# Splitting the first batch's queries and keys straight from PSUM, on ScalarE and VectorE

## What is computed

```python
def _attn_ref(q, k, v, n_sink, window):          # q, k, v: (2, 8, 768, 64), n_sink 4, window 128
    scores = 1.0 / np.sqrt(D) * np.matmul(q, k.transpose(0, 1, 3, 2))
    keep = (pos[None, :] < n_sink) | ((rel >= 0) & (rel < window))
    scores = np.where(keep, scores, -1000000000.0)
    a = np.exp(scores - np.max(scores, axis=-1, keepdims=True))
    a = a / (np.sum(a, axis=-1, keepdims=True) + 1e-09)
    return np.matmul(a, v)

def _moe_ref(x, U, V, w_ch1, w_ch2):             # rank 32, 512 -> 2048 -> 512
    u = x + (x.transpose(0, 2, 1) @ U @ V).transpose(0, 2, 1)
    return u + np.maximum(u @ w_ch1, 0.0) @ w_ch2

def _moe2_ref(x, w_tok1, w_tok2, w_ch1, w_ch2):  # 768 -> 256 -> 768, 512 -> 1536 -> 512
    u = x + (np.maximum(x.transpose(0, 2, 1) @ w_tok1, 0.0) @ w_tok2).transpose(0, 2, 1)
    return u + np.maximum(u @ w_ch1, 0.0) @ w_ch2
```

## Time and profile before

| | |
|---|---|
| median of three runs | 656.0 us (655.68 to 656.14) |
| the profiled execution | 657.41 us |
| its span, first to last instruction | 655.6 us |
| around the span | 1.8 us |
| PE busy | 631.2 us, 96% of the span |
| GpSimd busy | 367.0 us, 56% |
| DVE busy | 336.7 us, 51% |
| ACT busy | 316.2 us, 48% |
| attention of batch 0 | 3.9 us to about 77 us |

### The profile page before, as it was taken

One profiled execution on the slowest core, in us unless ns is written; L12 is line 12 of the kernel. 1 busy time (PEld: TensorE's weight loads), 2 busy tenths in 40 slices (PEclk: granted clock), 3 DMA queues, 4 the chain that ended last, 5 costly groups with the idle time before them and its releaser, 6 DMA issues.

```text
span 655.6 us, 10345 instructions
## 1 busy us (share of the span) xinstructions
PE 631.2 (96%) x3532; PEld 565.9 (86%) x3532; DVE 336.7 (51%) x733; ACT 316.2 (48%) x707; POOL 367.0 (56%) x373
## 2 busy tenths in 40 slices
PE   6888999999999999999999999999999999999998
PEld 5878888889888987799999988889998888899986
DVE  7776552433333254276757562186758325676411
ACT  4655575455444553464545444364544445554321
POOL 8544366656464656246656745375656543757262
PEclk9998999999999999999999999999999999999999
DMA  8344244433324425223232243233232343431142
GB/s 182 85 93 113 50 129 118 110 102 108 97 67 107 148 65 146 64 67 110 81 106 88 70 135 101 81 112 97 81 108 87 103 136 98 134 94 47 49 130 95
DMA packets 88276, 65.51 MB, mean 100 GB/s; under 512 B 43008, under 2 KB 72192, under 8 KB 88224
## 3 DMA queue, kind: packets, MB, share of 16 engines
q1 hardware_dynamic: 88224, 64.85, 35.0%
HBM read 61.42 MB, written 3.15 MB: 98 GB/s over the span
## 4 chain that ended last, share of the span: by engine, by line
PE 87%; DVE 5%; ACT 3%; POOL 2%; issue 2%; DMA 0%; DVEq 0%; ACTq 0%; POOLq 0%
PE bank L1356 33%; PE bank L1155 21%; PE bank L1322 10%; PE bank L1212 4%; PE bank L1185 4%; PE bank L1193 3%; PE bank L1286 3%; PE bank L1249 2%; PE bank L1230 2%; PE bank L1170 1%; PE bank L1263 1%; POOL w_lo L753 1%; ACT w_hi L774 1%; PE bank L1348 1%; DVE x_nat L978 1%
## 5 line engine op out<-in xcount | busy, mean ns | idle before, releaser
L753 POOL TENSOR_TENSOR w_lo<-w_raw,w_hi 128x512 fp32r<-128x512 f32 (+1 forms) x158 | 205.9, 1309 | 170.5 <-ACT w_hi L774 170.0
L774 ACT ACTIVATE w_hi<-w_raw 128x512 fp32r<-128x512 f32 (+1 forms) x158 | 96.3, 618 | 61.0 <-PE bank L1356 43.0
L1155 PE MATMUL bank<-b_hi,a_hi 128*128 128x384 f32 x280 | 94.8, 338 | 1.0 <-DVE temps L1065 0.6
L1155 PE MATMUL bank<-b_lo,a_hi 128*128 128x384 f32 x280 | 94.8, 339 | 0.0
L1356 PE MATMUL bank<-w_hi,hid_hi 128*128 128x512 f32 x216 | 87.6, 406 | 0.0
L800 ACT ACTIVATE probs<-masked,neg_max 128x264 f32<-128x264 f32 x96 | 49.5, 516 | 74.3 <-DVE neg_max L951 73.8
L1356 PE MATMUL bank<-w_hi,hid_lo 128*128 128x512 f32 x216 | 85.1, 394 | 0.0
L1356 PE MATMUL bank<-w_lo,hid_hi 128*128 128x512 f32 x216 | 84.7, 392 | 0.0
L1356 PE MATMUL bank<-w_hi,y_hid 128*128 128x512 f32 x216 | 71.1, 394 | 0.2
L951 DVE CUSTOM_DVE_ANT_0 masked<-bank,masks 128x264 f32<-128x264 f32 x96 | 41.2, 430 | 39.4 <-PE bank L1185 35.5
L718 POOL COPY p_sink<-probs 128x12 f32<-128x12 f32 x96 | 19.3, 202 | 69.8 <-ACT probs L800 68.2
(11 more groups left out here) (137 smaller groups left out, 1410.0 us busy)
## 6 DMA issues: line engine op xcount, KB each, us to landing
w_raw<-in_moe_w_ch_dram SPq DMA_DIRECT2D x144, 256.0 KB, 2.7
w_raw<-in_moe_w_ch_dram SPq DMA_DIRECT2D x20, 512.0 KB, 3.5
q_nat<-in_q_dram SPq DMA_DIRECT2D x12, 256.0 KB, 3.0
k_nat<-in_k_dram SPq DMA_DIRECT2D x12, 256.0 KB, 3.7
v_nat<-in_v_dram SPq DMA_DIRECT2D x12, 256.0 KB, 3.4
out_dram<-o_stage SPq DMA_DIRECT2D x12, 256.0 KB, 3.6
w_raw<-in_moe_w_tok_dram SPq DMA_DIRECT2D x6, 256.0 KB, 2.7
w_raw<-in_moe_w_tok_dram SPq DMA_DIRECT2D x8, 192.0 KB, 2.3
```

The source lines that it names most:

```text
L753: nc.gpsimd.tensor_tensor(w_lo[:, split % NW, 0:n], w_raw[:, split % NR, 0:n], w_hi[:, split % NW, 0:n].bitcast(f32), ALU.subtract) \
L774: nc.scalar.activation(w_hi[:, split % NW, 0:n], w_raw[:, split % NR, 0:n], ACT.Copy) \
L1155: last = mm(bank[:, 0:HALF], w[at % 2][:, a, k, :], u[:, b_part, k, :], start=(first and n == 0), stop=(n == 5), skip_group_check=True)
```

## The change

For tiles 0 to 5 of batch 0 there is no full copy of queries and keys any more. ACT writes the high parts straight from the PSUM bank (one instruction for the queries, two for the keys, four for the keys of tile 0 with their sinks), and DVE makes the low parts from the same bank and the high parts (one instruction and two). GpSimd has no part in it. The bank is now free for the next transposes only when the low parts are made: `wait_drained` waits for `q_split` and `k_split` instead of `q_copied` and `k_copied`. In the plan, `kT` goes from h = 2 to h = 3; `qsplit` goes behind the other steps of h = 0, and the whole of `ksplit` behind those of h = 3. Tiles of batch 1 are prepared as before, the first of them (T = 6, during tile 5) too.

```diff
             if u == 0:
                 now += [("qT", T), ("kT", T), ("qsplit", T), ("ksplit", T)]
...
-            if u < hi and T + 1 < NTILES:
+            if b == 0 and T + 1 < NQ:
+                if h == 0:
+                    now.append(("qT", T + 1))
+                    after.append(("qsplit", T + 1))
+                if h == 3:
+                    now.append(("kT", T + 1))
+                    after.append(("ksplit", T + 1))
+            elif u < hi and T + 1 < NTILES:
...
-            now += scores + pv + probsT
+            now += scores + pv + probsT + after
...
-                src = k_full[rows, :, :]
+                src = by_pair(tp_banks[tp_bank_of["kT", T]])[rows] if T < NQ else k_full[rows, :, :]
...
         def query_low(eng, T):
+            if T < NQ:
+                eng.scalar_tensor_tensor(out=q_lo[:, T % 2, :, :], in0=by_pair(tp_banks[tp_bank_of["qT", T]]),
+                                         scalar=-SCALE, in1=q_hi[:, T % 2, :, :].bitcast(f32),
+                                         op0=ALU.mult, op1=ALU.subtract).then_inc(q_split, 1)
+                return
...
-            if kind == "qT":
-                eng.wait_ge(q_copied, at + 1)
+            if kind == "qT" and at < NQ:
+                eng.wait_ge(q_split, at + 1)
+            elif kind == "kT" and at < NQ:
+                eng.wait_ge(k_split, keys_split(at))
...
-                elif s[0] == "qsplit" and s[1]:
+                elif s[0] == "qsplit" and s[1] >= NQ:
                     pool.wait_ge(q_high, s[1] + 1)
                     query_low(nc.gpsimd, s[1])
-                elif s[0] in ("ksplit", "ksplit_odd") and s[1]:
+                elif s[0] in ("ksplit", "ksplit_odd") and s[1] >= NQ:
...
+                if s[0] == "qT" and s[1] < NQ:
+                    T = s[1]
+                    act.wait_ge(tp_ready, tp_at[s] + 1)
+                    if T >= 2:
+                        act.wait_ge(scores_ready, H * (T - 1))
+                    nc.scalar.activation(q_hi[:, T % 2, :, :], by_pair(tp_banks[tp_bank_of[s]]),
+                                         ACT.Copy, scale=-SCALE).then_inc(q_high, 1)
+                elif s[0] == "kT" and s[1] < NQ:
+                    T = s[1]
+                    act.wait_ge(khi_zeroed, 2)
+                    act.wait_ge(tp_ready, tp_at[s] + 1)
+                    if T >= 2:
+                        act.wait_ge(scores_ready, H * (T - 1))
+                    for src, dst, sinks, sink_dst in key_parts(k_hi, T):
+                        if T == 0:
+                            nc.scalar.activation(sink_dst, sinks, ACT.Copy)
+                        last = nc.scalar.activation(dst, src, ACT.Copy)
+                    last.then_inc(k_high, 1)
...
-                    dve.wait_ge(q_copied, T + 1)
-                    if T >= 2:
+                    if T < NQ:
+                        dve.wait_ge(q_high, T + 1)
+                        query_low(nc.vector, T)
+                    else:
+                        dve.wait_ge(q_copied, T - NQ + 1)
                         dve.wait_ge(scores_ready, H * (T - 1))
-                    nc.vector.tensor_copy(q_hi[:, T % 2, :, :], q_full).then_inc(q_high, 1)
...
-                    dve.wait_ge(k_copied, T + 1)
-                    dve.wait_ge(khi_zeroed, 2)
...
+                    if T < NQ:
+                        dve.wait_ge(k_high, T + 1)
+                        if T == 0:
+                            dve.wait_ge(klo_zeroed, 2)
                         for e in range(2):
                             key_low(nc.vector, lambda sem, n: None, T, e)
```

More of the change, by code:

```diff
@@ L71, in attention @@
             now, scores, probsT, pv = [], [], [], []
+            after = []
             if u == 0:
@@ L785, in _ @@
                     T = s[1]
-                    if T:
+                    if T > NQ:
                         act.wait_ge(k_split, keys_split(T - 1))
@@ L915, in _ @@
                     T = s[1]
-                    dve.wait_ge(q_copied, T + 1)
-                    if T >= 2:
+                    if T < NQ:
[3 more added lines that the diff above has]
+                        dve.wait_ge(q_copied, T - NQ + 1)
                         dve.wait_ge(scores_ready, H * (T - 1))
-                    nc.vector.tensor_copy(q_hi[:, T % 2, :, :], q_full).then_inc(q_high, 1)
-                    if T == 0:
-                        dve.wait_ge(q_high, 1)
-                        query_low(nc.vector, T)
+                        nc.vector.tensor_copy(q_hi[:, T % 2, :, :], q_full).then_inc(q_high, 1)
                 elif s[0] == "ksplit":
                     T = s[1]
-                    dve.wait_ge(k_copied, T + 1)
-                    dve.wait_ge(khi_zeroed, 2)
-                    if T % NQ == 0 and T:
-                        dve.wait_ge(scores_ready, H * T)
-                    elif T >= 2:
-                        dve.wait_ge(scores_ready, H * (T - 1))
-                    for src, dst, sinks, sink_dst in key_parts(k_hi, T):
-                        if T % NQ == 0:
-                            nc.vector.tensor_copy(sink_dst, sinks)
-                        last = nc.vector.tensor_copy(dst, src)
-                    last.then_inc(k_high, 1)
-                    if T == 0:
-                        dve.wait_ge(k_high, 1)
-                        dve.wait_ge(klo_zeroed, 2)
+                    if T < NQ:
+                        dve.wait_ge(k_high, T + 1)
+                        if T == 0:
+                            dve.wait_ge(klo_zeroed, 2)
                         for e in range(2):
                             key_low(nc.vector, lambda sem, n: None, T, e)
+                    else:
+                        dve.wait_ge(k_copied, T - NQ + 1)
+                        dve.wait_ge(scores_ready, H * T if T == NQ else H * (T - 1))
+                        for src, dst, sinks, sink_dst in key_parts(k_hi, T):
+                            if T == NQ:
+                                nc.vector.tensor_copy(sink_dst, sinks)
+                            last = nc.vector.tensor_copy(dst, src)
+                        last.then_inc(k_high, 1)
                 elif s[0] == "scores":
```

9 lines of the change are left out of this document (5 added, 4 removed).

## The result

The changed kernel takes **660.98 us** (median of six runs, 660.89 to 662.16), the kernel before 656.3 (six runs, 655.68 to 657.28: the three of the table above and three more). The ratio is 1.0074, with a 95% interval of 1.0061 to 1.0087: slower by 0.74%. The prediction had the direction of its likeliest chance right (slower), and was 4 us too low; the result lies above the range of 654.0 to 659.4.

What follows compares the result with a forecast made beforehand. It took batch 0's attention as bound by engines waiting for each other, not by any engine's amount of work. From the median 656.0, waits + 2.7 and a held clock - 1.7 gave 657.0 us, range 654.0 to 659.4.

Steps and rivals of the forecast that it cites:

- The base of the sum: Tile 3: PE's half-clock stretch of some 3 us would not occur, - 1.7 us, taken from the median.
- first rival: PE's clock falls in tile 3 as before, so 656.0 + 2.7 = 658.7 us; chance 0.22.
- The waits: Tiles 0 to 4, batch 0: PE's waits change by 0.5 + 0.84 + 3 x 0.44 = + 2.7 us.
- The hand-over of a bank from DVE to PE: Tile 2: PE's transposes start 0.05 us after DVE frees the bank, as from 2.67 to 2.72.
- Two instructions on different halves of the partitions: Keys' split, tile 2: ACT's second instruction starts 0.49 us behind the first; DVE's pair takes 0.61 + 0.69.
- the replay: Tile 2 followed step by step with durations from the profile: `down` at 9.23 against 8.79, 0.44 us longer.
- The start: Tile 0: PE's first scores at 8.44 instead of 9.08 us; with later waits + 0.5, between - 0.6 and + 1.6.
- The mechanism: Tiles 2 to 4: `sums_eps` shortens by 1.01 us, but PE newly waits 0.54 us for queries' and 0.76 for keys' bank.
- The price of the low parts: DVE's low part of 512 elements from PSUM takes 0.69 us, as from SBUF.
- the third rival: Each PSUM read by DVE's low parts costs 0.065 us more: 658.0 us; chance 0.05.
- The second rival: DVE's low parts run at the pace of its casts, banks free earlier, `down` at 8.59: 653.8 us; chance 0.17.
- the fourth rival: One more clock fall in another tile besides tile 3's, + 1.7: 660.4 us; chance 0.08.

Runs made afterwards that it cites:

- same_rows: Changed kernel with the odd heads' keys read and written on the same 64 partitions as the even heads' (same amount of work): 660.53 us, one execution.
- klow_quarter: Changed kernel with DVE's low parts of batch 0's keys over 32 of 128 columns per pair of heads, the rest left out: 656.67 us, one execution.
- order_only: Kernel before with only the change's new places in the plan; full copies and GpSimd's part stay: 659.51 us, ratio 1.0042.
- sums_early: Kernel before with `sums_eps` and the reciprocal moved ahead of the split of the sink values (h = 3): 652.92 us, ratio 0.9940.
- after_old_order: Changed kernel with the key transposes and the split of the keys back in h = 2: 665.51 us, ratio 1.0141.
- late_and_early: Kernel before with `sums_eps` and reciprocal ahead of the sink values' split, and batch 0's key split behind h = 5: 653.13 us, ratio 0.9944.

## Why the prediction was wrong

The number was 657.0, the result 660.98. Two steps failed, and they add up.

**The base of the sum: 1.7 us.** This step is the subtraction of a held clock from the median. "The profiled execution is 1.8 us longer than its span and 1.4 above the median, which does not touch the difference" was the wrong sentence. The profiled execution stood above the median because the clock had fallen in it, and that fall was what I subtracted. From the median only what the median contains may be subtracted: 656.0 + 2.7 = 658.7, the number of my first rival, for the other reason. The size was off as well, 1.23 us instead of 1.67: I compared tile 3 with tile 2, and what is left of the difference is other work of tile 3.

**The waits: 4.9 us instead of 2.7.** Together with the base this closes the account: 657.0 + 1.7 + 2.2 = 660.9. By stretches, predicted and measured against the baseline without a fall (for tile 0 from the first transposes at 3.89 in both to the start of tile 1: 12.87 us before, 13.38 after):

| | predicted | measured |
|---|---|---|
| tile 0 | + 0.5 | + 0.5 |
| tile 1 | + 0.84 | + 1.44 |
| tile 2 | + 0.44 | + 0.92 |
| tile 3 | + 0.44 | + 0.94 |
| tile 4 | + 0.44 | + 1.14 |
| sum | + 2.7 | + 4.9 |

Where the 0.48 us of tile 2 are, term by term, with t from the start of the tile:

- *The hand-over of a bank from DVE to PE.* I took 0.05 us from the end of DVE's instruction to the start of the transposes. It is 0.14 to 0.15 in all three places (32.80 to 32.94, 34.80 to 34.95, 38.29 to 38.44). The trace of before had the number: ACT's copy that ended at 18.12 let the transposes go at 18.26. Three times 0.09 is 0.27, of which the queries' part shows as 2.78 instead of 2.72 and the key transposes stand at 4.79 instead of 4.64.
- *Two instructions on different halves of the partitions.* I let them overlap, by rows of instructions that are on all 128. ACT's pair took 1.19 us instead of 1.08, DVE's 1.41 instead of 1.30; `same_rows` gives 1.07 and 1.28. That is 0.2 us a tile by these terms; the experiment has 0.36 in tile 2, and 1.6 us by the start of tile 5, tile 0 included.
- The rest of the replay held: which waits there are and in which order, the scores of unit 19 0.38 us behind the key transposes (predicted 0.36), and the distance from the last wait to `down`, 1.43 us against 1.41.

In tile 1 the same two terms account for some 0.4 of the 0.6 us too little, by estimate (two hand-overs and the two pairs). The rest begins with a wait of 0.93 us of the sinks for GpSimd's `p_sink` (22.14), where the kernel before has one of 0.79 for ACT's copy; I had not followed that place closely. In tile 4 `x_nat` starts 0.24 us after DVE was free, and PE waits 0.25 for it (the same wait, 0.26, stands in tile 4 of `klow_quarter`). No such gap is in tile 2, and what makes it stays open.

**What was right.** The start: PE's first scores at 8.38 us, predicted 8.44 (9.08 before), and the gain lost again to a wait of 1.37 us for tile 1's keys; tile 0 came out at the predicted + 0.5, which with a range of 2.2 us is in part luck. The mechanism: `sums_eps` at 0.17 us in every tile, the wait for `x_nat` gone, transposes that wait for `q_lo` and `k_lo`, at 0.45 and 0.89 us near the "0.5 and 0.8" of the text. The price of the low parts: 0.684 us for `q_lo` and 0.687 for `k_lo` from PSUM, where I had taken 0.69 from `x_nat` and from `k_lo` in SBUF. The groups by shape of the first 80 us (busy us, mean ns):

```profile
L514 DVE TENSOR_TENSOR k_lo<-bank,k_hi 64x512 fp32r<-64x512 f32 x12 | 8.2, 687 | 2.2 <-ACT k_hi L810 2.1
...
L499 DVE SCALAR_TENSOR_TENSOR q_lo<-bank,q_hi 128x512 fp32r<-128x512 f32 x6 | 4.1, 684 | 1.5 <-ACT q_hi L799 1.5
```

So the third rival, by which each read of PSUM costs 0.065 us more, is out: the table of the Trainium skill ("VectorE: DVE Perf Modes", the section on the TRN2 errata, 120 fixed cycles against 58) is not borne out by these rows. The second rival, low parts at the pace of casts, is out by the same rows. The clock in 51 to 54 us is at full in the profiled execution, as said, but that was in part luck: another of the six executions of the changed kernel has a mean clock of 0.997. Nor was the fourth rival right, though its 660.4 lies nearest to the result: it has a fall of the clock in its sum, and the profiled execution has none.

**Why it lost, in one sentence.** The change gained the 1.0 us of stretched `sums_eps` in each of tiles 2 to 4, which could be had by moving two small instructions, and paid for it in every tile by doing 3.5 us of serial work of three engines in a bank that PE wants again within two units.

## What to carry to other kernels

Before a step moves from SBUF to PSUM, write down who wants that bank next and how much work the waiting engine has until then; what the hold is longer than that turns into a wait, and a shorter hold came back nearly in full (0.80 us less gave 0.79). Then count the other waits of the tile, since a wait moved to another place can take another's place (1.95 us instead of 0.89 made a tile 0.1 us longer). And before a total is read as the price of a wait, look at the clock in each tile. When a small instruction is stretched by another engine, first try to move the small one: here that brought 0.6%, and removing the other engine's work cost 0.7%. Before a difference is taken off a median, ask whether it is in the median at all: a profile is one execution.

## What the runs showed of the hardware that I had not expected

- The clock of PE falls in some executions of the same program and not in others, at different waits (tile 3 in one, behind tile 5 in another), to 0.50 for 3 to 4 us, and one fall cost 1.23 us where it could be read. Most of the falls in the profiled executions begin during a wait of PE or up to 0.7 us behind one; in `order_only` it is 2.2 us. All five runs of `sums_early` have a mean clock of 1.00, and all four of `after_old_order`, with waits of 2 us, 0.995 or less; but the profiled execution of `late_and_early`, whose last wait before it was 0.97 us, has a fall too. That the waits decide it was not tested by itself.
- A bank goes from DVE to PE's transposes in 0.14 to 0.15 us; the same from ACT (0.14).
- ScalarE, like DVE, does not overlap two instructions when they are on different halves of the partitions: 1.19 us for two of 0.59, against 1.07 on the same half.
- GpSimd's subtraction on SBUF holds `sums_eps` (SBUF to SBUF) to its own end, 1.18 us for 8 elements, and leaves `x_nat` beside it (PSUM and a small operand from SBUF) at 0.69. The cast of V from SBUF to SBUF takes 0.55 us alone, and 1.16 (`order_only`) or 0.95 (`sums_early`) where it starts beside GpSimd's subtraction.
- At the start of the program PE's products take as long as at half the clock (0.42 us for a score product, as at 27.10 in the fall of `after_old_order`), while the granted clock of the rows reads 1.00 there.
